# Attention and experts in one block, constants made inside it, the first head's maxima three banks at a time, the first gates ranked behind the first maximum

## The chip, the cores and the metric

One NeuronCore of one Trainium2 chip runs the kernel. Its engines are PE (TensorE), DVE (VectorE), ACT (ScalarE), POOL (GpSimd) and SP (SyncE), each with its own instruction stream; they meet only at semaphores and at the barriers between blocks. The metric is the device time of one execution in microseconds (us). The kernel before takes 1202.93 us, the median of three runs from 1200.16 to 1203.36.

## The reference

Three stages follow each other. The inputs are `q`, `k`, `v` of shape (4, 8, 1152, 64), a mixture of four small causal attention experts over 576 tokens of width 512, and a mixing layer with an MLP of width 2048.

```python
q_pool = q.reshape(B, H, S // 2, 2, D).mean(axis=3)        # 576 pooled queries per head
scores = D ** -0.5 * q_pool @ k.transpose(0, 1, 3, 2)      # 576 x 1152, for 32 heads
attn = exp(scores - max(scores)); attn /= sum(attn) + 1e-9
x = heads side by side of attn @ v                         # (4, 576, 512)

logits = x @ w_gate; the two largest of four experts, softmax of the two as weights
for e in range(4):
    a = causal softmax of (x @ wq[e]) @ (x @ wk[e]).T * Hd ** -0.5
    out += weight[e] * (a @ (x @ wv[e])) @ wo[e]

u = out + V.T @ (U.T @ out)                                # over the token axis
result = u + relu(u @ w_ch1) @ w_ch2
```

## The kernel before, in words

**Attention** (`attention`, one block of the program) goes head by head through 32 heads. For each head the scores are computed twice. A first pass finds the row maxima: queries on the partitions, keys in three pieces of 384 columns, five query tiles, so 15 pieces (`PIECES`). Each piece is one matmul into one of two PSUM banks used in turn (`max_piece` on PE, line 339) and one reduction on DVE (`max_piece`, line 600); DVE's `maximum` (line 606) joins the 15 partial maxima and writes them, negated, beside the low part of the queries. PE turns that tile (`turn_q_lo_m`, the transpose helper's line 298), ACT copies it out (`copy_q_lo_m`, line 515), and only then can the second pass finish a score tile (`score`, lines 349 and 358), whose result ACT takes through the exponential (`exponent`, line 529). POOL and DVE add up the exponentials, PE multiplies them with `v` (`values`, line 372).

The order on each engine is written out by hand. In the loop over heads, the maxima of head h+1 stand between the score tiles of head h. Only head 0's maxima have nothing beside them: they stand before the loop. ACT prepares keys and queries of a head (`cast_keys` line 483, `cast_queries` line 490) well before they are turned; for head 2 the two casts stand before the copies of head 1's turned keys.

SP issues all loads. For head 0 they are `k_raw`, then the two parts of `q_raw` (lines 181, 183, 186); one semaphore (`kq_loaded`) counts all three, and ACT's first cast waits for the whole count.

Before the attention block stands a small block of its own, in which POOL makes the identity matrix in three steps (lines 1757 to 1763). After it stands a block with the experts. The end of a block is a barrier over all engines.

**Experts** (`experts`): for each batch, 20 steps of score tile, mask and maximum on DVE (`maximum`, lines 1470 and 1474), exponential on ACT (line 1351), scaling on POOL (line 1088), turning on PE (line 1190), with projections for the next expert in between (`FILL`). The first batch's projections (`START`) already stand in the last head of the attention block. The last of these, for DVE, is `rank_gates` (lines 1430 to 1441), which ranks the four gate logits; ACT exponentiates its result (line 1365), and DVE's `weigh_gates` (lines 1447 to 1453) finishes the gates. DVE's program of the expert block begins with a memset of a padding (line 1505).

**MLP** (`mlp`): a block of its own, unchanged here.

## Time and profile before

| | before |
|---|---|
| median of 3 runs | 1202.93 us (1200.16 to 1203.36) |
| profiled execution | 1200.94 us, its span 1199.2 us |
| PE busy | 1141.5 us, 95% of the span |
| DVE, ACT, POOL busy | 650.0, 543.9, 521.9 us |
| before PE's first matmul | 8.2 us |
| attention without its first head's maxima | 24.8 to 533.3 us |
| from PE's last matmul of the attention block to its first of the experts' | 2.8 us |
| MLP | 784 to 1199.2 us |

The span runs from the first instruction to the last; 1.7 us of the execution lie outside it. A time in a row is counted from the span's start. "Idle before" in brackets is how long the engine had nothing to do before that row and what released it. PE is busy nearly everywhere, so the stretches in which it is not are what a reader looks for: the first 25 us and the place where one block ends and the next begins.

### The profile page before, as it was taken

To read this page: it belongs to the slowest core of one execution; us is meant where nothing else is said; L and a number is where in the kernel's file an instruction comes from. 1 tells how busy PE (TensorE), PEld (TensorE's weight loads), DVE (VectorE), ACT (ScalarE), POOL (GpSimd) and SP (SyncE) were. 2 spreads that over 40 slices of the span, in tenths; PEclk is the share of its full clock that TensorE was granted. 3 is DMA by queue.
4 is the path that set the end of the run, shared out by engine and by line. 5 is a ranking of instruction groups with operands and counts; after the bars stand their busy time and mean duration, and the time that the engine had idled before them with its cause. 6 is when DMAs were issued, how large, how long until landed. Compare 5 with 4: busy or idle time off the path is not lost. (4 is left out here: it accounts for less than half of the span.)

```text
span 1199.2 us, 19574 instructions
## 1 busy us (share of the span) xinstructions
PE 1141.5 (95%) x7232; PEld 956.5 (80%) x7232; DVE 650.0 (54%) x1380; ACT 543.9 (45%) x1131; POOL 521.9 (44%) x560
## 2 busy tenths in 40 slices
PE   6999999989999999998899999789999999999998
PEld 4777777777778777777777777579898989899896
DVE  4788877767888888856556565554121212122120
ACT  4666665565666666546565656633020201111010
POOL 5788899998888888734333333200000000000000
PEclk9999999999999999998999999989999999999999
DMA  8111112211122111003001010132100101010000
GB/s 203 50 54 51 57 60 60 60 43 49 60 60 61 60 60 40 21 1 141 1 1 41 1 41 27 41 123 84 53 1 15 39 1 52 0 52 0 27 1 27
DMA packets 47559, 54.56 MB, mean 46 GB/s; under 512 B 10992, under 2 KB 29424, under 8 KB 46960
## 3 DMA queue, kind: packets, MB, share of 16 engines
q1 hardware_dynamic: 47472, 53.42, 14.3%
q8 instruction: 53, 0.87, 0.3%
q14 instruction: 34, 0.28, 0.1%
HBM read 43.97 MB, written 9.44 MB: 45 GB/s over the span
## 5 line engine op out<-in xcount | busy, mean ns | idle before, releaser
L600 DVE TENSOR_REDUCE part_max<-psA 128x1 f32<-128x384 f32 x480 | 258.4, 556 | 67.9 <-PE psA L339 46.8
L529 ACT ACTIVATE pT<-psA 128x576 f32<-128x576 f32 x288 | 187.7, 652 | 165.5 <-PE psA L358 156.4
L251 POOL TENSOR_TENSOR pT<-pT 128x576 f32<-128x576 f32 x157 | 225.0, 1433 | 25.8 <-ACT pT L529 4.0
L339 PE MATMUL psA<-kT,qT 128*128 128x384 f32 x480 | 174.5, 388 | 11.3 <-DVE part_max L600 10.9
L372 PE MATMUL psA<-pT,v_raw 128*64 128x288 f32 x1152 | 153.9, 412 | 0.0
L1706 ACT ACTIVATE hid_hi<-psC 128x384 fp32r<-128x384 f32 x96 | 47.2, 492 | 198.4 <-PE psC L1631 198.3
L349 PE MATMUL psA<-qT,kT 128*128 128x288 f32 x576 | 133.5, 314 | 0.0
L1725 DVE SCALAR_TENSOR_TENSOR hid_lo<-psC,hid_hi 128x384 fp32r<-128x384 f32 x96 | 53.5, 558 | 137.8 <-ACT hid_hi L1706 137.8
L358 PE MATMUL psA<-qTm,kT 128*128 128x288 f32 x576 | 124.1, 297 | 0.2 <-ACT qTm L515 0.2
L339 PEld LDWEIGHTS psA<-kT,qT 128*128 128x128 f32 x480 | 88.4, 193 | 40.0 <-DVE part_max L600 21.2
L372 PEld LDWEIGHTS psA<-pT,v_raw 128*64 128x64 f32 x1152 | 77.1, 137 | 53.1 <-issue 6.4
L349 PEld LDWEIGHTS psA<-qT,kT 128*128 128x128 f32 x576 | 99.2, 190 | 18.3 <-issue 14.0
L1647 PE MATMUL psC<-w_hi,hid_hi 128*128 128x512 f32 x288 | 113.7, 395 | 0.0
L1647 PE MATMUL psC<-w_hi,hid_lo 128*128 128x512 f32 x288 | 112.5, 391 | 0.0
L1647 PE MATMUL psC<-w_lo,hid_hi 128*128 128x512 f32 x288 | 112.3, 390 | 0.0
L358 PEld LDWEIGHTS psA<-qTm,kT 128*128 128x128 f32 x576 | 93.4, 191 | 0.5 <-issue 0.5
L1631 PE MATMUL psC<-uT_hi,w_hi 128*128 128x384 f32 x384 | 83.1, 339 | 1.4 <-DVE uT_lo L44 1.4
L1631 PE MATMUL psC<-uT_lo,w_hi 128*128 128x384 f32 x384 | 82.9, 338 | 0.0
L1631 PE MATMUL psC<-uT_hi,w_lo 128*128 128x384 f32 x384 | 82.3, 337 | 0.0
L1088 POOL TENSOR_SCALAR moe_probs<-moe_probs,moe_sum_inv,gate 128x128 f32<-128x128 f32 (+4 forms) x80 | 53.3, 666 | 65.3 <-DVE moe_sum_inv L1461 61.2
L1351 ACT ACTIVATE moe_probs<-psB,moe_neg_max 128x128 f32<-128x128 f32 (+4 forms) x80 | 45.5, 569 | 68.0 <-DVE moe_neg_max L1474 67.3
L1631 PEld LDWEIGHTS psC<-uT_hi,w_hi 128*128 128x128 f32 x384 | 68.6, 190 | 2.2 <-DVE uT_lo L44 1.8
(162 smaller groups left out, 1931.7 us busy)
## 6 DMA issues: line engine op xcount, KB each, us to landing
k_raw<-in_k SPq DMA_DIRECT2D x32, 288.0 KB, 2.9
v_raw<-in_v SPq DMA_DIRECT2D x32, 288.0 KB, 2.8
q_raw<-in_q SPq DMA_DIRECT2D x32, 256.0 KB, 3.2
w_raw<-in_moe_w_ch SPq DMA_DIRECT2D x1, 4096.0 KB, 14.0
u_rows<-x_all SPq DMA_DIRECT2D x16, 256.0 KB, 2.0
w_raw<-in_moe_w_ch SPq DMA_DIRECT2D x16, 256.0 KB, 2.7
u_first<-u_rows SPq DMA_DIRECT2D x3, 768.0 KB, 4.5
u_second<-u_rows SPq DMA_DIRECT2D x3, 768.0 KB, 4.8
```

Of the source, the lines that this page charges most:

```text
L251: nc.gpsimd.tensor_tensor(pT[:, KT, :], pT[:, KT, :], pT[:, j, :], ALU.add).then_inc(part_summed, 1)
L339: nc.tensor.matmul(maxes[n % 2][:, 0:PIECE], qT[h % 3][:, t * P:(t + 1) * P], kT[u][:, c * PIECE:(c + 1) * PIECE], start=True, stop=True). ...
L349: nc.tensor.matmul(out[:, half, 0:HALF], kT[u][:, j * P:(j + 1) * P], qT[h % 3][:, half * HALF:(half + 1) * HALF], start=True, stop=False)
L358: mm = nc.tensor.matmul(out[:, half, 0:HALF], kT1[u][:, j * P:(j + 1) * P], qTm[u][:, half * HALF:(half + 1) * HALF], start=False, stop=True)
L372: mm = nc.tensor.matmul(o_bank[half * D:(half + 1) * D, at:at + HALF], v_raw[u][:, j, :], pT[:, j, half * HALF:(half + 1) * HALF], start=( ...
L529: nc.scalar.activation(pT[:, j, :].rearrange("p (a c) -> p a c", a=2), scores[n % 2][:, :, 0:HALF], ACT.Exp, scale=0.5 * float(D) ** -0.5) ...
L600: nc.vector.tensor_reduce(part_max[u][:, t, c:c + 1], maxes[n % 2][:, 0:PIECE], AX.X, ALU.max).then_inc(max_freed[n % 2], 1)
L1088: nc.gpsimd.tensor_scalar(p, p, sum_inv[0:rows, e, i:i + 1], gate[b % 2][0:rows, i, e:e + 1], ALU.mult, ALU.mult).then_inc(scaled, 1)
L1631: mm = nc.tensor.matmul(up[f % 4], w1_s[w][:, k, f * P:(f + 1) * P], uT[x][:, k, :], start=((w, x, k) == (*PARTS3[0], 0)), stop=((w, x, k) ...
L1647: mm = nc.tensor.matmul(down[t], hid[h][:, f, t * P:(t + 1) * P], w2_s[w][:, f, :], start=(n == 0), stop=(n == 3 * FC - 1))
L1706: nc.scalar.activation(hid[0][:, f, :], up[f % 4], ACT.Relu).then_inc(up_hi, 1)
L1725: nc.vector.scalar_tensor_tensor(hid[1][:, f, :], up[f % 4], 0.0, hid[0][:, f, :].bitcast(F32), ALU.max, ALU.subtract).then_inc(up_lo, 1)
```

## The change

1. **Constants.** The block that made the identity matrix is gone. POOL makes it at the head of the attention block; PE waits for it (`constants_made`), and so does DVE before the three constants that it derives from it.
2. **First loads.** For head 0, ACT issues the two loads of `q_raw`, SP that of `k_raw` and then at once those of head 1. DVE's first work on the queries waits for the padding of `q_raw` alone (`queries_padded`), no longer for all paddings.
3. **First head's maxima.** The 15 pieces become 5 groups of three: for one query tile, PE fills three neighbouring banks (banks 0 to 2 or 3 to 5 in turn) and DVE reduces all three in one instruction, 128x3 from 128x3x384. They wait until all the keys have been copied. The first group of head 1's transposes stands before the fifth.
4. **Order on ACT and POOL at the start.** ACT's casts for head 2 move behind the copy of head 0's `q_lo_m`. POOL's copy of head 0's high keys moves ahead of one subtraction.
5. **One block.** Attention and experts share a block. Each engine waits for `x_ready` (the last head's output, 32) in place of the barrier.
6. **Gates.** DVE ranks the first batch's gates behind the first expert maximum instead of before it, and the padding of line 1505 (of the second key buffer) behind that.

```diff
@@ attention @@
+        def wide(t):
+            return psum[:, 3 * (t % 2) * BANK:3 * (t % 2 + 1) * BANK].rearrange(
+                "p (c k) -> p c k", c=3)[:, :, 0:PIECE]
...
-                sp.dma_start(q_raw[u][:, 0:QT - 1, :],
...
+                sp.dma_start(k_raw[u][:, :, :], k_v[:, h:h + 1, :, :]).then_inc(kq_loaded[u], 16)
+                if h > 0:
+                    load_q(sp, h)
...
+            sp.wait_ge(x_ready, HEADS)
+            ahead.sync(sp)
...
+            nc.gpsimd.memset(ident[:, :], 0.0).then_inc(made, 1)
...
+            nc.gpsimd.tensor_copy(ident_r[:, :], ident[:, :]).then_inc(made, 1)
...
             split_k_lo(pool, nc.gpsimd, 1)
+            copy_k_hi(0)
             split_q_lo(pool, nc.gpsimd, 1)
-            copy_k_hi(0)
...
+            pool.wait_ge(x_ready, HEADS)
+            ahead.gpsimd(pool)
...
+            def wide_maxima(t):
+                if t == 0:
+                    pe.wait_ge(qa_copied, 1)
+                    pe.wait_ge(turn_freed, keys_before["kc", 0] + 1)
+                if t >= 2:
+                    pe.wait_ge(wide_reduced, t - 1)
+                for c in range(3):
+                    mm = nc.tensor.matmul(wide(t)[:, c, :], qT[0][:, t * P:(t + 1) * P],
+                                          kT[0][:, c * PIECE:(c + 1) * PIECE],
+                                          start=True, stop=True)
+                mm.then_inc(wide_filled, 1)
...
-            pe.wait_ge(padded, PADS)
+            pe.wait_ge(made, 3)
...
-            for at in range(len(PIECES)):
-                max_piece(0, at)
+            for t in range(QT - 1):
+                wide_maxima(t)
             turn_keys(1, "ka", range(0, 4))
+            wide_maxima(QT - 1)
             turn_queries(1)
             turn_keys(1, "kb", range(4, 8))
+            pe.wait_ge(padded, PADS)
             turn_q_lo_m(0)
...
+            pe.wait_ge(x_ready, HEADS)
+            ahead.tensor(pe)
...
+            load_q(act, 0)
             for h in range(2):
                 cast_keys(h)
                 cast_queries(h)
...
+            copy_q_lo_m(0)
             cast_keys(2)
             cast_queries(2)
-            copy_keys(1, "ka")
-            copy_queries(1)
-            copy_keys(1, "kb")
-            copy_q_lo_m(0)
...
+            def wide_maxima(t):
+                dve.wait_ge(wide_filled, t + 1)
+                nc.vector.tensor_reduce(part_max[0][:, t, :], wide(t), AX.X, ALU.max
+                                        ).then_inc(wide_reduced, 1)
...
-            first(0, ("vg", 4))
+            dve.wait_ge(x_ready, HEADS)
+            ahead.vector(dve)
@@ experts, DVE @@
+                if n == 0:
+                    do(b, ("vg", QT - 1))
+                    pad_k_lo(1)
@@ build @@
-            with nc.Block() as block:
-                @block.sync
-                def _(sp):
-                    ahead.sync(sp)
...
```

Order on PE, first head's maxima, before (names: `kT`, `qT` turned keys and queries, `psA` PSUM):

```order
L298 MATMUL psA<-ident_r,k_parts 128x128 [waits keys_copied]
L298 MATMUL psA<-ident_r,q_hi 128x128
L339 MATMUL psA<-kT,qT 128x384 [waits keys_copied,queries_copied]
L339 MATMUL psA<-kT,qT 128x384
L339 MATMUL psA<-kT,qT 128x384 [waits max_freed0]
L339 MATMUL psA<-kT,qT 128x384 [waits max_freed1]
```

And now, down to the turning of the maxima:

```order
L367 MATMUL psA<-kT,qT 128x384 [waits keys_copied,queries_copied]
L367 MATMUL psA<-kT,qT 128x384 x5
L367 MATMUL psA<-kT,qT 128x384 [waits wide_maxima_reduced]
L367 MATMUL psA<-kT,qT 128x384 x2
L367 MATMUL psA<-kT,qT 128x384 [waits wide_maxima_reduced]
L367 MATMUL psA<-kT,qT 128x384 x2
L328 MATMUL psA<-ident_r,k_parts 128x128 [waits keys_copied,k_lo_split]
L328 MATMUL psA<-ident_r,k_parts 128x128 x3
L367 MATMUL psA<-kT,qT 128x384 [waits wide_maxima_reduced]
L367 MATMUL psA<-kT,qT 128x384 x2
```

Instead of a wait for a bank before each matmul from the third on, there are three waits, one per group from the third on, and head 1's first key transposes have moved ahead of the fifth group.

Order on ACT from head 1's casts to the first exponential, before:

```order
L483 ACTIVATE k_parts<-k_raw 128x9x64 [waits kq_loaded1]
L490 ACTIVATE q_hi<-q_pool 128x640 [waits pooled]
L483 ACTIVATE k_parts<-k_raw 128x9x64 [waits turn_filled,kq_loaded0]
L490 ACTIVATE q_hi<-q_pool 128x640 [waits queries_turned,pooled]
L503 ACTIVATE kT<-psA 128x512 [waits turn_filled]
L508 ACTIVATE qT<-psA 128x512 [waits queries_turned]
L503 ACTIVATE kT<-psA 128x512 [waits turn_filled]
L515 ACTIVATE qTm<-psA 128x512 [waits max_filled]
L515 ACTIVATE qTm<-psA 128x128 [waits max_filled]
L529 ACTIVATE pT<-psA 128x576 [waits scores_ready]
```

And now:

```order
L530 ACTIVATE k_parts<-k_raw 128x9x64 [waits kq_loaded1]
L537 ACTIVATE q_hi<-q_pool 128x640 [waits pooled]
L550 ACTIVATE kT<-psA 128x512 [waits turn_filled]
L555 ACTIVATE qT<-psA 128x512 [waits queries_turned]
L550 ACTIVATE kT<-psA 128x512 [waits turn_filled]
L562 ACTIVATE qTm<-psA 128x512 [waits max_filled]
L562 ACTIVATE qTm<-psA 128x128 [waits max_filled]
L530 ACTIVATE k_parts<-k_raw 128x9x64 [waits turn_filled,kq_loaded0]
L537 ACTIVATE q_hi<-q_pool 128x640 [waits queries_turned,pooled]
L576 ACTIVATE pT<-psA 128x576 [waits scores_ready]
```

The two casts of head 2 now stand directly before the first exponential.

Order on DVE where attention ends and the experts begin, before (`x_all` is attention's output, `later` and `minus` the causal mask):

```order
L653 TENSOR_TENSOR x_all<-psA,sum_inv 32x64 [waits full_tiles_written]
L1430 TENSOR_TENSOR beats<-vals0 128x80 [waits b_freed2,b_freed1,last_tiles_padded,b_made]
...
L1441 TENSOR_TENSOR below_top<-vals0,gate_sum 128x20 [waits b_dve_step]
L101 UNCONDITIONAL_BRANCH
L1802 UNCONDITIONAL_BRANCH [waits barrier_Pool_Activation_PE_DVE_SP_release]
L1505 MEMSET moe_kT1 64x576
L1470 COPY_PREDICATED psB<-later,minus 128x128 [waits b_scores_ready]
```

And now:

```order
L708 TENSOR_TENSOR x_all<-psA,sum_inv 32x64 [waits full_tiles_written]
L1529 COPY_PREDICATED psB<-later,minus 128x128 [waits x_ready,b_scores_ready]
L1533 TENSOR_REDUCE moe_neg_max<-psB 128x1 [waits masked]
L1489 TENSOR_TENSOR beats<-vals0 128x80 [waits b_freed2,b_freed1,last_tiles_padded,b_made]
...
L1500 TENSOR_TENSOR below_top<-vals0,gate_sum 128x20 [waits b_dve_step]
L1567 MEMSET moe_kT1 64x576
L1529 COPY_PREDICATED psB<-later,minus 128x128 [waits b_scores_ready]
```

The ranking and the padding now stand between the first and the second mask, and the two branches with the barrier are gone.

## Rows read from the trace of the kernel before

**Rows 1.** Windows by stage: length, busy us (instructions) per engine, granted clock, DMA share, GB/s

```profile
0.00:8.20 8.20, 0.00 (x0) 0.00 (x0) 3.11 (x12) 2.62 (x3) 5.14 (x11) 1.00 0.57 152
8.20:24.80 16.60, 13.61 (x48) 8.87 (x48) 8.20 (x17) 7.14 (x14) 6.96 (x7) 1.00 0.97 239
24.80:482.50 457.70, 448.14 (x3213) 354.87 (x3213) 366.21 (x747) 294.87 (x550) 391.67 (x316) 1.00 0.19 56
...
533.30:539.60 6.30, 3.52 (x31) 3.27 (x30) 2.85 (x15) 1.15 (x3) 0.28 (x1) 1.00 0.00 0
539.60:548.00 8.40, 6.58 (x34) 6.11 (x35) 5.44 (x18) 3.42 (x11) 2.60 (x12) 0.80 0.90 347
...
784.00:1199.20 415.20, 407.06 (x2088) 371.49 (x2088) 89.71 (x150) 66.59 (x130) 0.00 (x0) 0.99 0.10 34
```

**Rows 2.** Timeline, 0 to 8 us: start, length, engine, line, operation

```profile
0.73 0.20 POOL L1757 MEMSET ident<- 128x128 f32 x1 [0.29 <-POOLq L1819]
...
2.30 0.41 SPq L181 DMA_DIRECT2D k_raw<-in_k  x1
...
2.30 1.28 ACT L483 ACT_TABLE_LOAD   x1 [2.30 <-PEq L1754]
...
3.23 0.59 SPq L186 DMA_DIRECT2D q_raw<-in_q  x1
...
6.63 0.68 ACT L483 ACTIVATE k_parts<-k_raw 128x576 fp32r<-128x576 f32 x1 [3.05 <-DMA q_raw<-in_q]
```

**Rows 3.** Timeline, 11 to 29 us: first head's maxima and first scores

```profile
11.39 0.97 PE L339 MATMUL psA<-kT,qT 128*128 128x384 f32 x2
...
11.80 0.27 ACT L500 ACTIVATE kT<-psA 128x128 fp32r<-128x128 f32 x1
...
12.07 1.02 DVE L600 TENSOR_REDUCE part_max<-psA 128x1 f32<-128x384 f32 x2 [3.56 <-PE psA L339]
...
16.89 0.74 ACT L490 ACTIVATE q_hi<-q_pool 128x640 fp32r<-128x640 f32 x1 [2.74 <-POOL q_pool L212]
...
22.16 0.17 DVE L606 TENSOR_REDUCE q_lo_m<-part_max 128x5 fp32r<-128x15 f32 x1
...
23.23 0.84 PE L298 MATMUL psA<-ident_r,q_lo_m 128*128 128x128 f32 x5
...
23.97 0.77 ACT L515 ACTIVATE qTm<-psA 128x512 fp32r<-128x512 f32 x2
...
24.88 0.82 PE L358 MATMUL psA<-qTm,kT 128*128 128x288 f32 x2 [0.21 <-ACT qTm L515]
...
29.54 0.43 PE L358 MATMUL psA<-qTm,kT 128*128 128x288 f32 x2
```

**Rows 4.** Timeline, 540 to 549 us, DVE: reductions of other widths

```profile
540.52 0.29 DVE L1474 TENSOR_REDUCE moe_neg_max<-psB 128x1 f32<-128x128 f32 x1
...
548.13 0.69 DVE L1474 TENSOR_REDUCE moe_neg_max<-psB 128x1 f32<-128x512 f32 x1
```

**Rows 5.** Timeline, POOL alone, 22 to 60 us

```profile
35.88 3.00 POOL L251 TENSOR_TENSOR pT<-pT 128x576 f32<-128x576 f32 x2 [0.77 <-ACT pT L529]
```

**Rows 6.** Timeline, 533 to 548 us: attention ends, experts begin

```profile
536.52 0.20 DVE L653 TENSOR_TENSOR x_all<-psA,sum_inv 32x64 f32<-32x64 f32 x1
...
537.37 0.24 DVE L1430 TENSOR_TENSOR beats<-vals 128x80 f32<-128x80 f32 x1 [0.65 <-ACT vals L1339]
...
539.50 0.54 DVE L1505 MEMSET moe_kT<- 64x576 f32 x1 [0.47 <-PEq L101]
539.62 0.41 PE L1176 MATMUL psB<-moe_kT,moe_qT 128*128 128x128 f32 x2 [2.80 <-PEq L101]
...
543.20 0.30 DVE L1470 COPY_PREDICATED psB<-later,minus 128x128 f32<-128x128 int32 x1 [2.39 <-PE psB L1176]
...
547.64 0.33 PE L1190 MATMUL psB<-ident,moe_probs 128*128 128x128 f32 x1 [1.80 <-POOL moe_probs L1088]
```

**Rows 7.** Timeline, DVE alone, 28 to 100 us: head 1's join of maxima

```profile
38.09 0.17 DVE L606 TENSOR_REDUCE q_lo_m<-part_max 128x5 fp32r<-128x15 f32 x1
```

More of the change, by code:

```diff
@@ L97, in max_no @@
     def max_no(h, n):
-        return h * MAX_USES + n
+        return h * MAX_USES + n - len(PIECES)
     ctx = ExitStack()
@@ L593, in _ @@
             first(0, ("vg", 4))
+            act.wait_ge(x_ready, HEADS)
+            ahead.scalar(act)
         @block.vector
```

82 lines of the change are left out of this document (39 added, 43 removed).

## The prediction

> **What bounds the kernel now.** First come the windows by stage [rows 1]. In the heads from 24.8 to 482.5 us PE is busy for 448.14 of 457.70 us, in the MLP for 407.06 of 415.20 us: both are PE's, and no part of the change touches what is in them. What starts them earlier is worth its full length at the end. PE is not the bound in two stretches. Before 8.2 us it has no work, and until 24.8 us it is busy 13.61 of 16.60 us, at a pace that others set. From 533.3 to 539.6 us it is busy 3.52 of 6.30 us. The reader then follows each stretch in the timeline. At the start [rows 2] SP's first load goes out at 2.30 us, 1.57 us after POOL's first instruction of the identity's block; ACT's first cast waits for the loads until 6.63 us. In the first head's maxima [rows 3] DVE works from 12.07 to 22.16 us, 10.1 us for 15 pieces or 0.67 us each, where one reduction takes 0.51: with two banks in turn, PE and DVE wait for each other. The maxima are then turned at 23.23 us, 0.9 us after DVE's end at 22.33, since PE is still busy with head 1's keys. At the seam [rows 6] attention's last output is written at 536.72 us, yet PE starts its first expert score at 539.62 us, after 2.80 us of idling.
>
> **The change part by part.** Times are those of the profiled execution, 1200.94 us, which lies 1.99 us below the median of the three runs. The gains are summed there and taken off the median.
>
> Start: the identity's block and its barrier go. The first load then leaves where POOL's first memset left, at 0.73 instead of 2.30 us: 1.57 us earlier [rows 2]. The second part of head 0's queries went out 0.93 us after the first load and was the last to be waited for, 3.40 us after its own issue. As ACT's second issue it goes out some 0.45 us after the start, which could give 0.47 us more. Against that, head 1's keys now go out right behind head 0's and share the way. They are 0.295 MB; at the 239 GB/s of the next stretch [rows 1] that is 1.2 us if all of them pass first. So the ends are 1.57 - 1.2 = 0.4 and 1.57 + 0.47 = 2.0 us. I take 1.8, near the upper end, since the observed 3.40 us is mostly time to landing and the two queues hardly fill the engines so early. ACT's table load of 1.28 us now stands behind its two issues: 0.73 + 1.0 + 1.28 = 3.0 us, before the data lands at some 4.8 us, so it costs nothing. PE and DVE wait for the identity until about 1.9 us, as hidden.
>
> What that stretch bears on is also in the Trainium skill, "DMA: Bandwidth & Descriptors", section "Issuing engines are not separate DMA queues": loads from several engines run on the same 16 DMA engines and interleave, and only the issuing time is saved. By that rule the second issuer gives 0.47 us at most, and the 0.4 us end is a real one.
>
> Maxima: the five reductions of 128x1152 are in no row. Widths of 128 and 512 columns take 0.29 and 0.69 us [rows 4], so 1.04 ns a column and 0.16 us fixed; 1152 columns make 1.36 us, with 0.05 us to the next 1.41. The upper bound is three of today's 0.51 us reductions, 1.53 us [rows 3]. PE needs three matmuls of 384 columns. It runs at half speed here: the pair of line 358 takes 0.82 us at 24.88 and 0.43 us at 29.54 [rows 3], although the granted clock shows 1.00 for the stretch [rows 1]. At 1.2 GHz 384 columns are 0.32 us; the first result reached DVE 0.68 us after the matmul's start. A group is thus ready 0.64 + 0.68 = 1.32 us after PE may start. Two groups in turn allow one per (1.36 + 1.32 + 0.1)/2 = 1.39 us: DVE's 1.41 just decides. All keys must now be copied first, at 12.07 us, so DVE starts at 12.13 + 1.32 = 13.45 instead of 12.07, and ends at 13.45 + 5 x 1.41 = 20.5 instead of 22.16. Small maximum and hand-over make 20.8 us. PE has by then turned head 1's keys and queries, because the first transposes stand before the fifth group and ACT copies them meanwhile. The turning of the maxima thus starts at 20.8, not 23.23: 2.4 us gained, 1.7 with the upper bound of the reduction, and 2.5 if DVE were quicker still, because PE's 1.39 us then decides.
>
> The moved casts: ACT is free of `qTm` at 23.97 + 0.77 - 2.4 = 22.3 us and casts head 2 for 0.57 + 0.74 us, until 23.7. The first exponential could start at 24.88 + 0.82 - 2.4 = 23.3 us, so it is 0.4 us late. Queued behind the casts are the copies of head 1's last keys, the next exponentials and, on POOL, the subtraction for head 2 and the copy of head 1's keys, then its sums, 0.6 us late. PE has the second score tile and three maxima to do before it needs that exponential, and POOL idles 0.77 us within the first head's sums [rows 5]. I cost it at nothing; without that cover it is 0.6 us. Before, these casts lay in ACT's idle time (2.74 us before 16.89 [rows 3]). The reordered copy on POOL is free: PE asks for it only after turning the maxima.
>
> Seam: with the barrier gone PE waits only for `x_ready`, at 536.72, so its first score starts at 536.85 instead of 539.62. DVE masks and reduces it (0.5 us to its start, since PE's row is 0.41 us long, then 0.30 + 0.29 [rows 4, 6]) until about 538.05. Then it ranks the gates and writes the padding: 537.37 to 540.04 less 0.47 of idling is 2.2 us [rows 6]. The second mask starts at 540.3, against 543.20: 2.9 us earlier. PE's tile for it is ready at about 539, because the twelve projections of 288 columns ahead of it take 12 x 0.12 us at 2.4 GHz. Behind the ranking ACT waits with the gates' exponential and the copies of head 1 of the experts, ready at 539.8, and from there on DVE's string of work is the one of before. DVE bounds, not PE. The ends are 1.1 us (a 1.7 us price of the clock, see rivals) and 2.9 us; I take 2.8, nearest to the row of the idle itself. The 4 MB load of the MLP's weights moves with the start and only keeps its distance.
>
> Sum: 1.8 + 2.4 + 2.8 = 7.0 us. 1200.94 becomes 1193.9, and the median 1202.93 becomes 1195.9 us.
>
> **Rivals.**
>
> *The clock takes part of it back.* From 539.6 to 548.0 the granted clock averages 0.80 [rows 1]: 0.20 x 8.4 = 1.7 us lost in one stretch at 0.50, right after the 2.80 us of idling. That idling goes, but since DVE is the bound, PE idles longer before its first turning, 547.64, where it already waited 1.80 us [rows 6]: now about 2.6. If the clock falls there, 1.7 us are lost just where PE had dense work. At the start full speed came within 4 us of the first dense work; a stretch more at half speed costs another 1.7. Both together: 7.0 - 3.4 = 3.6 us gained, 1199.3.
>
> The Trainium skill, "TensorE: Matmul & The Clock Gate", section "HAM oscillation — how this bites in real kernels", says that waits of PE between groups of matmuls put the clock back to half, each time anew. By that rule the longer wait at the seam costs its 1.7 us and the sum is 5.3 us, 1197.6; the trace agrees for the 2.80 us gap and not for the one of 1.80.
>
> *Full speed comes earlier.* PE is busy for 0.96 of 1.41 us in the grouped maxima, against 0.64 of 1.34 before. If that is enough to raise the clock before the scores, some 4 us of dense work at 1.2 GHz take half: 2 us more, 1193.9. Against it: the denser transposes around 23 us did not raise it at once.
>
> *The loads come late.* Head 0's queries wait for head 1's keys: the start gives 0.4 instead of 1.8 us, total 5.6, 1197.3. For it speaks the DMA share of 0.97 from 8.2 us on; against it, that the share before is 0.57 [rows 1].
>
> *The change doesn't do what it says.* At the seam the barrier only gives way to waits of DVE, because ranking and padding now delay the second tile. If ACT's chain behind the gates is late too, 1.2 us are left of 2.8, total 5.4, 1197.5.
>
> *Slower.* The broken-up start keeps PE at half speed into the heads. A head takes some 16 us (the joins of two heads' maxima stand at 22.16 and 38.09 [rows 3, 7]) and is PE's, so at half speed it loses up to 16. To be slower by over 0.3% this must eat 7.0 + 3.6 = 10.6 us: from 21 us at half speed on. Two such heads' worth (32 us at half speed, 16 lost) give 1195.9 + 16 = 1211.9. Against it: once PE is dense, as before, the clock rose within 4 us.
>
> **How the numbers follow.** Forecast 0.50, own range 1194 to 1198; clock taking back 0.20; earlier full speed 0.10; late loads 0.07; seam replaced 0.10; slower 0.03. The predicted time is 1195.9 us. The range from 1191.5 to 1200.2 takes in the earlier clock at its best, the clock's price at both places and a run-to-run spread of 1.6 us on either side of the runs' middle. What a measurement can tell is 0.3%, 3.6 us: faster means below 1199.3. Half of the clock rival and a little of the others lie above it. Faster 0.86, same 0.11, slower 0.03.
>
> **What would show it.** The first load at about 0.7 us and ACT's first cast at 4.6 to 5.0 us; later than 5.5 means late loads. Five reductions of 128x3 from 128x1152 with 1.36 us each (1.53 or more is wrong) and 1.41 us between starts. The turning of the maxima 4.2 us earlier than before, 19.0 us, and the next join of maxima some 16 us after the first, as before. PE's wait before the first expert score under 0.3 us, the second mask 2.9 us earlier relative to attention's last output, and the granted clock near 1.00 in the four us after it. The MLP must take its 415.2 us unchanged. The forecast fails if the first heads take longer than before, or if the expert stage gives back at the clock what the seam gained.

## The result and the profile after

The changed kernel takes 1194.18 us (median of 5 runs, 1192.52 to 1196.58) against 1202.58 us (1200.16 to 1203.36) for the kernel before on the same chip: ratio 0.9946, 95% interval 0.9931 to 0.9961, 8.4 us. A word-for-word copy, run later beside others, gave 1196.89 against 1201.87: 0.9960 (0.9944 to 0.9977), 5.0 us. The copy's ten runs fall into four of 1193.3 to 1193.6 us with a mean granted clock of 0.992 or 0.993 and six of 1196.8 to 1198.9 us with 0.987 to 0.989, so a median moves with how many of each it holds. One comparison is therefore good to some 2 us, and the mean of the two, 6.7 us, lies by the 7.0 of the forecast. The profiled execution of the changed kernel took 1195.76 us with a span of 1194.0, 5.2 us less than the profiled one of before. Where these 5.2 us arise and go is told by places that both traces have:

| place | before | after | earlier by |
|---|---|---|---|
| first load issued | 2.30 | 0.73 | 1.57 |
| ACT's first cast | 6.63 | 5.51 | 1.12 |
| join of head 0's maxima | 22.16 | 19.50 | 2.66 |
| join of head 1's | 38.09 | 33.05 | 5.04 |
| join of head 2's | 53.42 | 50.24 | 3.18 |
| attention's last output | 536.52 | 533.56 | 2.96 |
| the experts' second mask | 543.20 | 537.33 | 5.87 |
| first turning of probabilities | 547.64 | 541.63 | 6.01 |
| second turning | 550.03 | 545.50 | 4.53 |
| MLP's first turning | 785.99 | 782.35 | 3.64 |
| end of the span | 1199.2 | 1194.0 | 5.2 |

Windows of the changed kernel's trace over the stretches of [rows 1]:

```profile
0.00:8.20 8.20, 1.07 (x8) 1.07 (x8) 3.67 (x12) 2.94 (x4) 5.80 (x12) 1.00 0.71 221
8.20:24.80 16.60, 13.24 (x68) 11.02 (x66) 9.22 (x11) 9.17 (x20) 7.44 (x8) 1.00 1.04 227
24.80:482.50 457.70, 446.24 (x3212) 352.62 (x3211) 368.73 (x748) 294.70 (x551) 394.05 (x318) 1.00 0.19 56
533.30:539.60 6.30, 5.52 (x37) 4.54 (x35) 5.10 (x23) 3.03 (x10) 1.59 (x9) 1.00 0.75 280
539.60:548.00 8.40, 6.37 (x38) 5.97 (x38) 5.65 (x15) 4.29 (x13) 4.25 (x10) 0.80 0.69 290
780.30:1194.00 413.70, 405.34 (x2089) 369.67 (x2088) 89.49 (x150) 66.53 (x130) 0.00 (x0) 1.00 0.10 33
```

PE has 1.07 us of work before 8.2 us, where it had none; from 24.8 to 482.5 us it is busy 1.9 us less than before, in a window of the same place and length, which points to a loss within the heads; in the 6.3 us at the seam it is busy 5.52 instead of 3.52 us.

The start, to be held against [rows 2]: ACT's queue now issues head 0's queries; the keys and head 1's loads go out from SP.

```profile
0.73 0.89 SPq L202 DMA_DIRECT2D k_raw<-in_k  x2
0.74 0.48 ACTq L189 DMA_DIRECT2D q_raw<-in_q  x1
...
1.25 0.54 ACTq L192 DMA_DIRECT2D q_raw<-in_q  x1
...
5.51 0.69 ACT L530 ACTIVATE k_parts<-k_raw 128x576 fp32r<-128x576 f32 x1 [2.40 <-DMA q_raw<-in_q]
```

The last queries are waited for from their issue at 1.25 to 5.51 us, 4.26 us, where it was 3.40 us before.

DVE's first maxima, to be held against [rows 3]:

```profile
12.44 2.62 DVE L652 TENSOR_REDUCE part_max<-psA 128x3 f32<-128x1152 f32 x2 [5.05 <-PE psA L367]
15.22 2.62 DVE L652 TENSOR_REDUCE part_max<-psA 128x3 f32<-128x1152 f32 x2 [0.16 <-PE psA L367]
18.03 1.36 DVE L652 TENSOR_REDUCE part_max<-psA 128x3 f32<-128x1152 f32 x1 [0.19 <-PE psA L367]
19.50 0.17 DVE L661 TENSOR_REDUCE q_lo_m<-part_max 128x5 fp32r<-128x15 f32 x1
```

The rows start 2.78 and 2.81 us apart with two reductions in each, so 1.4 us a reduction. The turning of these maxima by PE starts at 19.81 us and takes 0.60 us for what took 0.84 at 23.23 us [rows 3]; the next rows of PE are from the same timeline:

```profile
19.81 0.60 PE L328 MATMUL psA<-ident_r,q_lo_m 128*128 128x128 f32 x5 [0.85 <-DVE q_lo_m L661]
...
21.27 0.51 PE L401 MATMUL psA<-qTm,kT 128*128 128x288 f32 x2 [0.52 <-ACT qTm L562]
```

The two matmuls of 288 columns take 0.51 us instead of 0.82: PE already works at the higher of its two levels.

The loss within the heads. DVE, then POOL, then PE, each from its own timeline from 26 to 51 us:

```profile
33.05 0.17 DVE L661 TENSOR_REDUCE q_lo_m<-part_max 128x5 fp32r<-128x15 f32 x1
33.82 1.92 DVE L668 SCALAR_TENSOR_TENSOR p_sum<-pT 128x576 f32<-128x576 f32 x1 [0.59 <-ACT pT L576]
35.84 1.96 DVE L673 TENSOR_TENSOR p_sum<-p_sum,pT 128x576 f32<-128x576 f32 x1
...
50.24 0.17 DVE L661 TENSOR_REDUCE q_lo_m<-part_max 128x5 fp32r<-128x15 f32 x1
```

```profile
27.46 7.66 POOL L270 TENSOR_TENSOR pT<-pT 128x576 f32<-128x576 f32 x5
35.77 1.42 POOL L237 TENSOR_TENSOR k_parts<-k_raw,k_parts 128x576 fp32r<-128x576 f32 x1 [0.64 <-ACT k_parts L530]
```

```profile
39.92 0.44 PE L382 MATMUL psA<-kT,qT 128*128 128x384 f32 x1 [1.64 <-DVE part_max L647]
```

Two additions of DVE take 1.92 and 1.96 us where they take 0.74 to 0.76 us when POOL does nothing beside them. DVE's maxima for head 2 then come late, PE waits 1.64 us, and the joins of heads 1 and 2 lie 17.2 us apart instead of 15.3. The same rows show that POOL's additions run from 27.46 to 35.12 us without the idling of [rows 5].

The seam, to be held against [rows 6]:

```profile
533.56 0.20 DVE L708 TENSOR_TENSOR x_all<-psA,sum_inv 32x64 f32<-32x64 f32 x1
...
533.82 0.44 PE L1235 MATMUL psB<-moe_kT,moe_qT 128*128 128x128 f32 x2
...
537.33 0.27 DVE L1529 COPY_PREDICATED psB<-later,minus 128x128 f32<-128x128 int32 x1
...
541.63 0.48 PE L1249 MATMUL psB<-ident,moe_probs 128*128 128x128 f32 x1 [2.19 <-POOL moe_probs L1147]
...
545.50 0.38 PE L1249 MATMUL psB<-ident,moe_probs 128*128 128x128 f32 x2
```

PE's wait of 2.80 us before the first score is gone. Its wait before the first turning has grown from 1.80 to 2.19 us, and what lies between the first two turnings takes 3.87 us where it took 2.39.

### The profile page after: what moved, and what is told of

It is laid out like the page before. It is cut to its first block and busy times, and to the rows that moved or that the text cites. A ratio compares the mean times of both kernels' runs of the same rounds, so it can differ in the third digit from the quotient of the medians.

```text
span 1194.0 us, 19539 instructions
## 1 busy us (share of the span) xinstructions
PE 1135.8 (95%) x7232; PEld 951.8 (80%) x7232; DVE 651.6 (55%) x1370; ACT 543.9 (46%) x1131; POOL 523.4 (44%) x560
## 5 line engine op out<-in xcount | busy, mean ns | idle before, releaser
L647 DVE TENSOR_REDUCE part_max<-psA 128x1 f32<-128x384 f32 x465 | 250.6, 556 | 59.4 <-PE psA L382 36.7
L382 PE MATMUL psA<-kT,qT 128*128 128x384 f32 x465 | 166.0, 379 | 11.5 <-DVE part_max L647 11.1
L382 PEld LDWEIGHTS psA<-kT,qT 128*128 128x128 f32 x465 | 83.7, 189 | 36.5 <-DVE part_max L647 19.4
```

Source lines behind the costliest of these rows:

```text
L382: nc.tensor.matmul(maxes[n % 2][:, 0:PIECE], qT[h % 3][:, t * P:(t + 1) * P], kT[u][:, c * PIECE:(c + 1) * PIECE], start=True, stop=True). ...
L647: nc.vector.tensor_reduce(part_max[u][:, t, c:c + 1], maxes[n % 2][:, 0:PIECE], AX.X, ALU.max).then_inc(max_freed[n % 2], 1)
```

## The experiments

Ratios are to the kernel before on the same chip, with 95% intervals; single diffs are against the changed kernel unless another is named.

**The moved casts undone** (b1): ACT casts head 2 before it copies head 1, as before.

```diff
-                copy_keys(h, "ka")
-                copy_queries(h)
-                copy_keys(h, "kb")
                 if h == 0:
+                    copy_keys(0, "ka")
+                    copy_queries(0)
+                    copy_keys(0, "kb")
                     copy_keys(0, "kc")
-            copy_q_lo_m(0)
             cast_keys(2)
             cast_queries(2)
+            copy_keys(1, "ka")
+            copy_queries(1)
+            copy_keys(1, "kb")
+            copy_q_lo_m(0)
```

> The changed kernel, with one edit: ACT casts head 2's keys and queries before it copies head 1's turned keys, as in the kernel before. In the changed kernel the joins of the maxima of heads 1 and 2 stand 17.2 us apart (33.05 and 50.24) where 15.3 is the rule; DVE's two additions of exponentials take 1.92 and 1.96 us there instead of 0.76, beside POOL's late work, and PE then idles 1.64 us for a bank. Theory (moved casts make POOL late, and POOL beside DVE slows both): POOL starts head 0's additions at least 1.2 us earlier, DVE's two additions fall below 1.0 us each, the joins of heads 1 and 2 come to 15.3 to 15.6 us apart, and the time is 1.5 to 2 us below the changed kernel's 1194.2, about 1192.5. Rival (full clock from the start makes PE outrun POOL, whatever the order on ACT): the joins stay 17 us apart and the time stays at 1194.

0.9950 (0.9935 to 0.9964), no different from the changed kernel. POOL's split of head 2's keys moved from 21.77 to 15.96 us, yet its additions began at 26.50 us, not earlier (25.91 in the changed kernel). What kept POOL this time was the load of head 3's queries, for which it waited 1.60 us:

```profile
25.67 0.87 POOL L231 TENSOR_TENSOR q_pool<-q_raw 128x320 f32<-128x320 f32 x1 [1.60 <-DMA q_raw<-in_q]
```

Two signs of the theory did appear, joins 15.3 us apart (34.44 and 49.76) and one addition of 0.76 us, the other taking 1.14. But the granted clock was at half from 22.4 us on and the second join came late; the copy below shows the same joins with the casts moved. The place of the casts is worth nothing that can be measured, and drawing them forward did not make POOL's additions start earlier. What they would do in an execution with an early second join was not seen.

**Head 1's loads held back** (b2): SP waits until head 0's loads have landed.

```diff
             load_kq(0)
+            sp.wait_ge(kq_loaded[0], 48)
             load_kq(1)
```

> The changed kernel, with one edit: SP waits until head 0's keys and queries have landed before it issues head 1's loads. The changed kernel's first cast on ACT starts at 5.51 us, 4.26 us after the last of head 0's loads was issued, where it took 3.40 before. Theory (head 1's keys and queries share the DMA engines): the first cast starts at 4.7 us or earlier, and what hangs on it moves by 0.7 us or more, unless head 1's loads are now late. Rival (a second issuing engine has a slower way of its own): the first cast stays at 5.4 to 5.6 us. Time by the theory 1193.5, by the rival 1194.2.

The first cast came at 4.87 us, 0.64 us earlier than in the changed kernel. All other kernels with the new loads had it at 5.44 to 5.89 us, so sharing the way costs head 0 some 0.6 to 1.0 us. The whole took 0.9975 (0.9962 to 0.9989), 3 us more than the changed kernel. DVE and PE, 34 to 55 us, tell why:

```profile
34.69 0.17 DVE L662 TENSOR_REDUCE q_lo_m<-part_max 128x5 fp32r<-128x15 f32 x1
35.42 1.77 DVE L669 SCALAR_TENSOR_TENSOR p_sum<-pT 128x576 f32<-128x576 f32 x1 [0.56 <-ACT pT L577]
38.49 1.97 DVE L674 TENSOR_TENSOR p_sum<-p_sum,pT 128x576 f32<-128x576 f32 x1 [1.30 <-POOL pT L271]
...
42.58 0.44 PE L383 MATMUL psA<-kT,qT 128*128 128x384 f32 x1 [2.66 <-DVE part_max L648]
...
54.40 0.17 DVE L662 TENSOR_REDUCE q_lo_m<-part_max 128x5 fp32r<-128x15 f32 x1
```

All later loads are late with head 1's. POOL waits 3.42 us for head 3's queries, and its additions begin at 28.91 us:

```profile
28.09 0.86 POOL L232 TENSOR_TENSOR q_pool<-q_raw 128x320 f32<-128x320 f32 x1 [3.42 <-DMA q_raw<-in_q]
```

DVE then waits for POOL, its additions take more than twice their 0.76 us beside it, PE waits 2.66 us, and the joins lie 19.7 us apart. Right behind PE's wait, from 42.9 us, the granted clock was at 0.50 for 3.4 us, so up to 1.7 us of the loss is the clock's. Holding the loads back gained 0.6 us at the first cast, and attention's last output came at 537.55 us, 4.0 us later than in the changed kernel.

**Without the seam's part** (a2: the experts in a block of their own, gates ranked where they were; start and maxima changed) **and with one block, but the gates ahead of the first maximum** (a3):

```diff
 a2, on each of the five engines:
-            pe.wait_ge(x_ready, HEADS)
-            ahead.tensor(pe)
 a2 and a3:
+            first(0, ("vg", 4))
...
-                if n == 0:
-                    do(b, ("vg", QT - 1))
-                    pad_k_lo(1)
```

> The changed kernel with attention and experts in two blocks again and the gates ranked at the end of the first, as before: the first loads, the constants and the grouped maxima are kept. Theory (the seam is worth 2.9 us up to the experts' second mask, and the half clock that follows PE's longer idle time takes 1.5 us of it back): 1.4 to 2.9 us more than the changed kernel's 1194.2, so 1195.6 to 1197.1; PE idles 2.8 us at the seam. Rival (the whole of the 8.4 us gain is at the start): 1194.2, no difference.

> The changed kernel, one block kept, with the gates ranked on DVE ahead of the first expert maximum and the padding ahead of it too. DVE's work until the second mask is the same in sum, only its order differs. Theory (DVE's string of work bounds the seam, so its order hardly matters): the second mask starts within 0.3 us of the changed kernel's 3.57 us after attention's last output, and the time is within 0.5 us of 1194.2. Rival (ranking behind the first maximum is what makes the seam short): the second mask comes 1.5 to 2 us later and the time is 1196.

a2 0.9967 (0.9953 to 0.9981), a3 0.9968 (0.9953 to 0.9982). After attention's last output the second mask starts 7.09 us later in a2, 3.66 in a3 and 3.77 in the changed kernel (6.68 before). One block therefore brings the second mask forward whatever the gates' place; ranking behind the first maximum lets the fourth score start 5.15 instead of 5.78 us after the output, and the first turning 8.07 instead of 8.52 us after it. The times say something else. a3 took 1196.55 us, near the rival's 1196 and as long as a2 (1197.24), while b1, which differs from the changed kernel only in the casts, took 1195.15 us on that chip. Taken by themselves the times would give the gates' place the whole gain, but the intervals overlap. In a3's trace much of the delay lies away from the edit: attention's last output came at 535.39 us, after two falls of the granted clock in the heads (248.4 and 282.5 us) where the changed kernel had one, and 13.7 us from 777.5 us on were at half speed.

**The start alone** (a1: old maxima, casts, copy on POOL, blocks and gates) **and start with seam** (a4: old maxima, casts and copy). In both:

```diff
-            for t in range(QT - 1):
-                wide_maxima(t)
+            for at in range(len(PIECES)):
+                max_piece(0, at)
             turn_keys(1, "ka", range(0, 4))
-            wide_maxima(QT - 1)
```

> The start alone: constants made inside attention's block and head 0's queries loaded by ScalarE; 15 single reductions over two banks, the moved casts, the separate experts' block and the gates' place are as before. The loads shared with head 1's were seen to cost 0.6 us, so the start should give 1.1 us, not the 1.8 of the prediction: first cast at 5.5 us, first join of maxima at 21.0, ratio 0.999 (1201.5 against 1202.6). Rival (the start gives its full 1.8 us because what follows absorbs the late loads): join at 20.4, ratio 0.9985. Rival (a start moved by 1 us is lost again before the second head's join): second join at 38.1 as before, ratio 1.000.

> The changed kernel with the first head's maxima as before (15 reductions over two banks), the casts and GpSimd's copy at their old place too; start and seam as in the changed kernel. With the three others of the series it gives the price of the seam and the gates a second time, without the early clock of the changed start. Theory (the parts add up): the start alone measured 0.9996, seam and gates should add 2.8 us less 1.7 us that the clock takes: ratio 0.9986 to 0.9988, 1200.8. If the seam were worth its full 2.8: 0.9973. Rival (the seam's gain is given back wholly, as attention's output arrives at another time): 0.9996.

a1 0.9996 (0.9981 to 1.0012): first join at 21.20 us (0.96 earlier than before), second at 37.43 (0.66), output at 535.85 (0.67). a4 0.9967 (0.9953 to 0.9982), better than expected, though in its trace the start brought nothing: first join at 21.50, second at 38.17, output at 536.71 us. With the four corners the parts can be read twice each: the maxima give 0.0029 (a1 to a2) and 0.0014 (a4 to the mean of the changed kernel and its copy, 0.9953), the seam 0.0029 (a1 to a4) and 0.0014 (a2 to that mean). That is 3.5 and 1.7 us for each, 2.6 on average, each of them uncertain by some 2 us. What is called the maxima here includes the moved casts and POOL's copy. The start gives 0.5 us, not safely different from nothing.

**One tile at a time over six banks** (b3):

```diff
                 for c in range(3):
-                    mm = nc.tensor.matmul(...)
-                mm.then_inc(wide_filled, 1)
+                    if t >= 2: pe.wait_ge(wide_reduced, 3 * t + c - 5)
+                    nc.tensor.matmul(...).then_inc(wide_filled, 1)
```

> The changed kernel, but over its six banks VectorE reduces one 128x384 tile at a time: 15 reductions instead of 5. It separates the two things that the three-bank groups do at once: TensorE no longer waits for a bank, and VectorE issues a third of the instructions. Theory (VectorE's instruction count decides): 15 reductions 0.51 to 0.52 us apart take 7.8 us, against 7.0 in the changed kernel; they start 0.7 us earlier since one matmul is enough for the first, so the join of maxima comes at 19.5, the same, and the time is that of the changed kernel within 0.1%. Rival (each single reduction still waits for its matmul at half speed, 0.67 us as before): 10 us, join at 21.8, 2.3 us slower. Either way the result says what of the 2.4 us belongs to banks and what to fewer instructions.

DVE, 8 to 20 us:

```profile
12.01 7.06 DVE L652 TENSOR_REDUCE part_max<-psA 128x1 f32<-128x384 f32 x15 [4.42 <-PE psA L367]
19.18 0.17 DVE L661 TENSOR_REDUCE q_lo_m<-part_max 128x5 fp32r<-128x15 f32 x1
```

Fifteen reductions in 7.06 us, 0.47 us each and without a gap: the same as five wide ones in 6.95 us (12.44 to 19.39). (DVE's side of the edit is the same: each bank is reduced alone and freed at once.) The join is 0.3 us earlier, the time 0.9957 (0.9941 to 0.9973). With the old two banks the same 15 took 10.1 us. The gain of the maxima is that PE and DVE no longer wait for each other at two banks; that DVE issues a third of the instructions gives nothing.

**The copy** (c0: no edit) **and the first head's additions ahead of the pooling of head 3's queries on POOL** (c2):

```diff
+                if h == 0:
+                    add_tiles(0)
                 if h + 3 < HEADS:
                     pool_queries(pool, nc.gpsimd, h + 3)
-                add_tiles(h)
+                if h > 0:
+                    add_tiles(h)
```

> The changed kernel once more, word for word, so that the kernels beside it are compared with it on one chip, and to see how far the places named in the first trace repeat. Expected of both theories: ratio to the kernel before 0.9935 to 0.9955. Theory A (in the second head's start VectorE's and GpSimd's work on the same memory slows each other): if the first head's turning of maxima again runs at full speed, the two additions of lines 668 and 673 again take 1.9 us each and the second join of maxima stands at 33.0; if it runs at half speed, they take 0.76 to 1.1 us. Rival B (the 1.9 us were a disturbance of that one execution): additions of 0.76 us and a second join at 32.0 or earlier.

> The changed kernel with one GpSimd instruction moved: in the first head, the pooling of head 3's queries (line 231, 0.85 us) goes behind that head's additions of probability tiles instead of ahead of them. Theory A (GpSimd is the bound there: its additions ran without a gap from 27.46 to 35.12 us and VectorE's two additions beside it took 1.9 us each): the additions begin 0.85 us earlier, the overlap shrinks, VectorE's two take 0.8 to 1.4 us, and the second join of maxima comes 0.8 to 2 us earlier than in the copy of the changed kernel, of which TensorE's clock may take half: 0.05 to 0.15% faster. Rival (TensorE sets the second join): the join does not move, same time within 0.05%.

DVE of c0, then of c2, 33 to 51 us:

```profile
34.63 0.17 DVE L661 TENSOR_REDUCE q_lo_m<-part_max 128x5 fp32r<-128x15 f32 x1
35.37 0.76 DVE L668 SCALAR_TENSOR_TENSOR p_sum<-pT 128x576 f32<-128x576 f32 x1 [0.57 <-ACT pT L576]
...
49.95 0.17 DVE L661 TENSOR_REDUCE q_lo_m<-part_max 128x5 fp32r<-128x15 f32 x1
```

```profile
33.23 0.17 DVE L664 TENSOR_REDUCE q_lo_m<-part_max 128x5 fp32r<-128x15 f32 x1
33.99 1.08 DVE L671 SCALAR_TENSOR_TENSOR p_sum<-pT 128x576 f32<-128x576 f32 x1 [0.59 <-ACT pT L579]
35.18 1.24 DVE L676 TENSOR_TENSOR p_sum<-p_sum,pT 128x576 f32<-128x576 f32 x1
...
48.86 0.17 DVE L664 TENSOR_REDUCE q_lo_m<-part_max 128x5 fp32r<-128x15 f32 x1
```

In c0 the turning ran at full speed too (0.59 us), and still the 1.9 us that theory A asked for in that case did not come. From 21.6 to 25.0 us the granted clock was at 0.50, and PE reached the second join 1.6 us later than in the first trace, when POOL was nearly done: additions of 0.76 us, joins 15.3 us apart, and a third join within 0.3 us of the other trace's. In c2 PE was early and POOL 0.86 us earlier than in the copy: additions of 1.08 and 1.24 us, no wait of PE, and the third join 1.1 us before the copy's; attention's last output came at 532.34 instead of 533.37 us. The time, 0.9953 (0.9932 to 0.9975), is the same within what can be told.

**Without POOL's additions** (c1: the five later ones of head 0 cut to 64 columns; the sums of its other columns are left out).

> The changed kernel with GpSimd's five later additions of the first head cut from 576 to 64 columns; the sums of the first head's other columns are left out. Theory A (VectorE's two additions take 1.9 instead of 0.76 us, and GpSimd's 1.4 instead of 0.9, because the two engines work on the memory at the same time): with GpSimd done early the two additions take 0.76 us each even where the join before them comes early, no TensorE wait on part_max of over 0.5 us is left near 40 us, and the second join stands at 32.9 to 33.2 with the next one 15.3 to 15.6 us behind it. Rival (the two additions are slow for another reason, as transfers of the second and third heads' values): 1.1 us or more remain.

The clock fell again from 21 to 25 us, the second join stood at 34.74 us, and the additions took 0.76 us, as in c0 with POOL's work whole. The early join that the run needed did not occur, so by itself it decides nothing; the ends of the rows in the other traces decide (below).

**Work in PE's wait** (e1): the third expert's projection is done once more, ahead of the first turning.

```diff
                 elif kind == "p":
+                    if use == ("p", 0, 0) and b == 0:
+                        project_qk(b, 2, 0, False)
                     turn_probs(b, use[1], use[2])
```

> The changed kernel with useless work in TensorE's 2.19 us wait before the experts' first turning of probabilities: the twelve matmuls of the third expert's first projection (line 1217, 128x288) are done there a first time, and again at their own place. Nothing else is moved, and the output stays whole. In every trace so far the granted clock fell to half for 3.4 us (1.7 us of work lost) right behind that wait or behind the one before it. Theory A (the wait is what costs the clock): the wait shrinks to 0.1 us, the clock stays at 1.00 through 545, the second turning comes 3.9 to 4.0 us after the first output of attention's end is counted, that is 1.5 to 1.9 us earlier than in the changed kernel relative to attention's last output (11.94 us there), and the time falls by 1.7 us: 0.9940 against 0.9955. Rival B (the clock falls anyway, from the change of work and not from the wait): half speed somewhere within 540 to 548 as before, and the doubled work costs nothing or up to 2.1 us at the place: same or up to 0.15% slower.

Windows of two us (busy time by engine, granted clock, DMA share, GB/s), 540 to 546 us, first of the copy, then of e1:

```profile
540.00:542.00 2.00, 0.56 (x2) 0.50 (x3) 1.89 (x7) 0.67 (x2) 1.10 (x3) 0.60 1.02 434
542.00:544.00 2.00, 2.00 (x9) 1.65 (x8) 1.51 (x3) 0.95 (x3) 0.58 (x3) 0.50 0.99 418
544.00:546.00 2.00, 2.00 (x11) 1.98 (x10) 0.16 (x2) 0.83 (x2) 1.44 (x2) 0.50 0.62 258
```

```profile
540.00:542.00 2.00, 1.38 (x11) 1.15 (x10) 1.92 (x7) 0.67 (x2) 1.01 (x4) 1.00 1.00 426
542.00:544.00 2.00, 2.00 (x17) 1.81 (x16) 1.76 (x4) 1.05 (x4) 0.78 (x3) 1.00 1.02 434
544.00:546.00 2.00, 2.00 (x18) 2.00 (x17) 1.28 (x4) 1.96 (x7) 1.52 (x3) 1.00 0.78 324
```

PE of e1 at the two turnings:

```profile
541.73 0.33 PE L1250 MATMUL psB<-ident,moe_probs 128*128 128x128 f32 x1 [0.62 <-POOL moe_probs L1147]
...
544.12 0.38 PE L1250 MATMUL psB<-ident,moe_probs 128*128 128x128 f32 x2
```

The wait is 0.62 us instead of 2.19, the clock stays at 1.00 up to 774 us, and the second turning comes 10.46 us after attention's last output (533.66), against 11.94 us: 1.5 us. With twelve matmuls more, the kernel took 0.9942 (0.9919 to 0.9965), which is not told apart from the changed kernel. The gain is shown at its place only.

How much of the expert stage the clock decides is seen from attention's last output to the MLP's first turning:

| trace | half speed begins at (up to 770 us, 3.4 us each) | output to MLP's first turning |
|---|---|---|
| e1 | none | 244.20 |
| c2 | 541.8 | 246.20 |
| a3 | 545.4 | 246.45 |
| d2 | 549.6, 583.7 | 247.13 |
| changed | 541.5, 551.7, 585.9 | 248.79 |
| b1 | 541.2, 551.4, 585.6 | 248.80 |
| a2, two blocks | 535.8, 552.9, 587.0 | 250.66 |

All seven have one more stretch at half speed, of 3.4 to 13.7 us, that begins 3.9 to 5.4 us before the MLP's first turning. The 4.6 us between e1 and the changed kernel are thus not all the filler's. 1.5 us arise at the filled wait; the rest goes with the two later falls, which c2, without any filler, did not have either. Compared at three falls each, two blocks (a2) take 1.9 us more than one (changed, b1); at one fall each, the gates ahead (a3) take 0.25 us more than the gates behind (c2).

**All three together** (d2: six banks, POOL's additions first, work in the wait).

> The changed kernel with the three edits that looked good by themselves: single reductions over six banks in the first head, that head's additions on GpSimd ahead of the pooling of head 3's queries, and the twelve repeated matmuls in TensorE's wait before the experts' first turning of probabilities. Theory (each edit removes time at its own place: 0.5 us of the maxima, 0.9 us of GpSimd's additions, 1.7 us of the clock at the seam): attention's last output at 532.0 instead of 533.4 to 533.7, granted clock 1.00 from 532 to 560, the second turning of the experts' probabilities 10.5 us after that output, and a ratio of 0.993 to 0.9935. Rival (only the work in the wait is real, the other two are within the spread): 0.994, with the output at 533.4 or later.

1192.20 us (1191.04 to 1192.76) against 1199.86: 0.9935 (0.9922 to 0.9949), the lowest ratio of all; its interval still overlaps that of the changed kernel. The output came at 532.31 us and the second turning 10.45 us behind it, as in e1. But PE's next wait, 1.68 us before the fifth turning, was followed by a fall that e1 did not have. From the fifth turning to the next (548.00 to 553.15 us) it took 5.15 us, against 3.59 us in e1:

```profile
546.00:548.00 2.00, 0.32 (x2) 0.03 (x1) 1.68 (x5) 1.39 (x4) 1.43 (x4) 1.00 0.00 0
548.00:550.00 2.00, 1.88 (x12) 1.21 (x13) 1.25 (x4) 1.00 (x3) 0.83 (x3) 0.89 0.00 0
550.00:552.00 2.00, 2.00 (x9) 1.90 (x8) 1.62 (x4) 0.94 (x3) 1.22 (x3) 0.50 0.00 0
```

## Why the prediction was right, and where not

The forecast of 7.0 us held: 8.4 and 5.0 us in the two comparisons. Its terms did less well than their sum, and that the sum came out so near is in part luck. By the experiments' times the start gave 0.5 us instead of 1.8, the maxima 2.6 and the seam 2.6, each uncertain by some 2 us. In the two traces a gain that the sum did not have (2.4 us from the first join to the second, by the earlier full speed) and 1.5 us in the MLP stand against losses that it had put at nothing (1.9 us from the second join to the third, 1.5 us at the turnings).

*Start: 1.8 us, measured 1.1.* The load went out 1.57 us earlier as said, and the first cast came at 5.51 us, just past the 5.5 us that the text named as the mark of late loads. Head 1's transfers share the way (0.64 us against b2), so the truth lay in the middle of the two ends, 0.4 and 2.0. In the heads 0.7 us of it were left (a1).

*Maxima: 2.4 us, held.* Taking away the shift of the start, DVE was to start 1.38 us later than before and start its reductions 1.41 us apart; it started 12.44 + 1.12 - 12.07 = 1.49 us later and they stood 1.40 us apart. The turning came at 19.81 instead of 19.0 us because the start had given 0.7 us less. (The lower end of this term should read 1.6, not 1.7: five times 0.17 us off 2.4.) The working leaned on wide reductions of 1.36 us, which was right, but b3 shows that they are not what matters: it is the three tiles in flight, over six banks.

*Moved casts at nothing: right, for a cover that wasn't there.* The text leaned on POOL's 0.77 us of idling. With the first join 2.7 us earlier, POOL has no idling in the changed kernel's first head; it became the last one there. In b1 the casts at their old place changed nothing that could be measured. What the step missed is POOL's own chain. Head 1 arrived 5.0 us early and head 2 only 3.2.

The mechanism can be read off the ends of the rows. In the first heads, ten additions of 128x576 on DVE took longer than 0.76 us, and all ten ended 0.61 or 0.62 us after the end of an operation of POOL, whenever they had themselves begun:

| kernel | DVE's addition | POOL's operation ends | DVE ends | behind it |
|---|---|---|---|---|
| changed | 33.82, 1.92 | 35.12 | 35.74 | 0.62 |
| changed | 35.84, 1.96 | 37.19 | 37.80 | 0.61 |
| a2 | 34.99, 1.05 | 35.42 | 36.04 | 0.62 |
| b1 | 35.20, 1.14 | 35.72 | 36.34 | 0.62 |
| b2 | 35.42, 1.77 | 36.57 | 37.19 | 0.62 |
| b2 | 38.49, 1.97 | 39.85 | 40.46 | 0.61 |
| b3 | 34.87, 1.31 | 35.57 | 36.18 | 0.61 |
| c2 | 33.99, 1.08 | 34.46 | 35.07 | 0.61 |
| c2 | 35.18, 1.24 | 35.81 | 36.42 | 0.61 |
| d2 | 34.60, 1.47 | 35.45 | 36.07 | 0.62 |

In d2 POOL's addition had only 0.03 us left when DVE's began, and it is the end of POOL's next operation that counts.

The whole traces say the same. In the 14 together, 406 such additions met an operation of POOL that had more than 0.16 us left, and all ended 0.60 to 0.63 us behind its end. Of the 86 that met one with less left, 85 took the 0.75 to 0.77 us that they take anyway; the other is d2's. One kind of operation is different: 56 additions, four in each trace, met POOL's scaling of weights (`TENSOR_SCALAR` of 128x256) and ended 0.13 to 0.17 us behind it, after 0.95 us at most; why stays open.

So the engine that comes second does not work slowly; it stands until the first has finished. The other way round it holds too. POOL in c2, 30 to 40 us:

```profile
29.91 4.55 POOL L270 TENSOR_TENSOR pT<-pT 128x576 f32<-128x576 f32 x3
34.42 1.39 POOL L231 TENSOR_TENSOR q_pool<-q_raw 128x320 f32<-128x320 f32 x1
```

The pooling, 0.87 us long elsewhere, began while DVE's addition was in progress (until 35.07) and ended 0.74 us behind it. It is one of 17 operations of this size in the 14 traces that did so (0.72 to 0.74 us), and 115 of 128x576, 1.42 us long alone, ended 1.26 to 1.29 us behind DVE's addition.

The Trainium skill states this rule: "SBUF — State Buffer", section "SBUF: two separate sides", says that DVE and GpSimd share one pair of ports as an exclusive lock for a whole instruction, a DVE operation with two SBUF inputs included where GpSimd's reads SBUF. The traces agree for the 406 meetings above, and not for the 56 with the scaling. The section was not weighed in the forecast, and should have been: the trace of before has 28 such meetings too, the longest in line 618 at 280.91 us with 1.96 us. DVE's maxima of 128x384 read PSUM and pass untouched, with 0.55 or 0.56 us beside a two-input operation of POOL (272 in the changed kernel's trace) and without one (193), so only the sums suffer. c2, which moves POOL 0.86 us ahead, shortens the meeting and removes PE's wait.

*"Full speed comes earlier", a rival at 0.10.* It did, and in the changed kernel the second join followed the first by 13.55 us instead of 15.93. Of the eleven kernels with three tiles in flight, seven turned the first maxima in 0.59 or 0.60 us, the others in 0.85. It brought little that lasted. In five of the seven the clock was at half once more for 3.4 us between 20 and 26 us, and in the changed kernel DVE and POOL took it back: a2, at half speed there, has its last output at 532.61 us, the changed kernel at 533.56. From the third join to the last a head takes 15.72 to 15.79 us on average in all traces, so what is lost by the third join is not won back.

*Seam: 2.8 us, held at its place.* The first score followed the output by 0.26 us, and the second mask came 6.68 - 3.77 = 2.9 us earlier relative to it. Some of this is the clock's: in the trace of before, DVE waited 2.39 us for PE's second score [rows 6] while PE ran at half speed from 540.4 us on, and the three traces with the old seam have the second mask 6.24, 6.68 and 7.09 us after the output (a1, before, a2), which makes it 2.5 to 3.3 us. The timed part is 1.7 or 3.5 us. That the barrier counts for more than the gates' place is seen in the traces (a3 at the second mask, and the table under e1); the times alone do not show it.

*The clock takes it back, a rival at 0.20: it did, by 1.5 us, at the second of the two waits.* The granted clock stayed at 1.00 in the six us after the output, as the forecast asked. The rival named the first turning, and there the fall is. Before the change the half speed from 540.4 to 543.8 us fell on work that a wait of 1.80 us follows, which took up at least part of the loss; no trace of the old seam is without such a fall, so how much is not shown. In the changed kernel it lies behind the first turning, where no wait follows until the second: the two turnings lie 3.87 us apart instead of 2.39, and 6.01 us of lead became 4.53. The old seam is not safe from this either: a1 had a fall behind its first turning too, and 3.95 us between the turnings. That the wait brings the fall is shown by filling it. In the nine traces of one block without filler the clock falls 7.0 to 10.0 us after attention's last output, every time; in the two with filler (e1, d2) it does not, and both have the second turning 10.45 or 10.46 us after the output.

*The MLP "must take its 415.2 us unchanged": 413.7.* Its first twelve turnings of 128 columns take 2.67 us before and 1.50 us after, by the level of the clock they meet; that alone is 1.2 us. Over the 14 traces the MLP takes 411.0 to 414.3 us from its first turning to the end, by how long the clock is at half in it, so this part of the 5.2 us is not the change's.

## What to carry to other kernels

A stretch that a bank pair paces is read from the gaps in both engines' rows; more buffers in flight cured it here, and wider instructions added nothing. When the bound engine gets earlier, look at which engine has no idling left, here POOL, and whether its operations now meet DVE's, which then stand for their whole length. And ask of a removed wait where the next one is: half speed cost 1.5 us here where TensorE's work was dense and no wait followed, so harmless filler in the wait ahead of dense work can pay. Here it did so in the traces, by 1.5 us; in the times it could not be told from the spread.

## What was not expected of the hardware

- Fifteen reductions of 128x384 from PSUM in a row take 0.47 us each, and five of 128x1152 1.36 us or 1.31 in pairs: there is next to no fixed price to save.
- DVE's additions of 128x576 in SBUF ended 0.60 to 0.63 us behind the operation that POOL had running, in 406 cases (0.76 us alone, up to 1.97 us so), but only 0.13 to 0.17 us behind its `TENSOR_SCALAR` of 128x256; in the heads' steady state, where the ends just meet, line 668 takes 0.93 us on average over 30.
- A wait of 2.19 us was followed by 3.4 us at half the clock in the changed kernel, and a wait of 1.68 or 1.69 us by such a fall in d2 and in the changed kernel but not in e1 or c2. The same wait does not always cost the clock; what decides it stays open.
